# Two parts of x against the high weights in one product of 512 columns

## The reference

```
h = x @ w_in;  g = h if h > 0 else exp(h) - 1;   x = g @ w_out      # layer 0
h = x @ w_in;  g = s * max(h, 0)**2 + b;         out = g @ w_out    # layer 1
```

## Time and profile before

| | |
|---|---|
| median of 3 runs | 738.39 us (738.21 to 739.23) |
| profiled execution | 738.77 us |
| its span, first to last instruction | 736.9 us |
| PE busy | 99% of the span |
| PE weight loads | 90% |
| DVE busy | 75% |
| ACT busy | 68% |
| POOL busy | 67% |
| granted TensorE clock, mean | 0.999 |

### The profile page before, as it was taken

The page is one execution under the profiler, slowest core; times in us unless marked ns, Lnnn a source line. Parts: engine busy times, 40 slices in busy tenths (PEclk is TensorE's granted clock), DMA queues, the critical chain, the costliest instruction groups (busy, mean ns, idle before and its releaser), DMA issues.

```text
span 736.9 us, 14171 instructions
## 1 busy us (share of the span) xinstructions
PE 728.1 (99%) x4617; PEld 666.1 (90%) x4617; DVE 556.4 (75%) x1185; ACT 501.6 (68%) x941; POOL 496.5 (67%) x436
## 2 busy tenths in 40 slices
PE   8999999999999999999999999999999999999998
PEld 5999999999999889988998899989998999899986
DVE  6888888888888887877666777677767776766764
ACT  7888888888885767575657666577566656474552
POOL 6678899999998687835654577677655454644340
PEclk9999999999999999999999999999999999999999
DMA  5686765665524222321112223132112211131101
GB/s 167 160 177 134 162 169 138 156 170 123 136 61 107 86 89 85 115 58 58 31 56 59 61 88 110 58 95 85 52 57 78 78 47 58 58 102 43 58 1 57
DMA packets 78287, 67.82 MB, mean 92 GB/s; under 512 B 9284, under 2 KB 66964, under 8 KB 78228
## 3 DMA queue, kind: packets, MB, share of 16 engines
q1 hardware_dynamic: 77940, 66.80, 33.6%
q10 hardware_dynamic: 288, 0.26, 0.1%
HBM read 46.23 MB, written 3.19 MB: 67 GB/s over the span
## 4 chain that ended last, share of the span: by engine, by line
PE 79%; POOL 9%; DMA 4%; issue 4%; ACT 2%; DVE 2%; SPq 0%; POOLq 0%; DVEq 0%; ACTq 0%
PE acc L939 35%; PE h_ps L919 32%; PE pt_ps L859 4%; PE pv_ps L874 2%; PE pv_ps L875 2%; PE s_ps L845 2%; PE s_ps L846 2%; POOL pt_lo L562 2%; DMA x_parts<-x_second 2%; POOL qqk L550 1%; POOL pt_hi L560 1%; DMA qqk<-qqk 1%; POOL x L578 1%; POOL x_sum L569 1%; DMA qqk<-bits 1%
## 5 line engine op out<-in xcount | busy, mean ns | idle before, releaser
L624 POOL TENSOR_TENSOR wi_lo<-w_raw,wi_hi 128x512 fp32r<-128x512 f32 x96 | 98.8, 1030 | 188.6 <-ACT wi_hi L1035 186.0
L919 PE MATMUL h_ps<-xb_hi,wi_hi 128*128 128x256 f32 x672 | 190.2, 283 | 0.5 <-DVE u_sb L1362 0.5
L919 PE MATMUL h_ps<-xb_hi,wi_lo 128*128 128x256 f32 x672 | 190.2, 283 | 0.0
L919 PE MATMUL h_ps<-xb_lo,wi_hi 128*128 128x256 f32 x672 | 190.2, 283 | 0.0
L919 PEld LDWEIGHTS h_ps<-xb_hi,wi_hi 128*128 128x128 f32 x672 | 128.8, 192 | 2.6 <-DVE u_sb L1362 0.7
L919 PEld LDWEIGHTS h_ps<-xb_lo,wi_hi 128*128 128x128 f32 x672 | 128.8, 192 | 1.8
L919 PEld LDWEIGHTS h_ps<-xb_hi,wi_lo 128*128 128x128 f32 x672 | 128.8, 192 | 0.0
L629 POOL TENSOR_TENSOR wi_lo<-wi_sum,wi_hi 128x512 fp32r<-128x512 f32 x96 | 122.6, 1298 | 1.9 <-ACT wi_hi L1035 1.9
L1157 ACT ACTIVATE r_sb<-h_sb 128x512 f32<-128x512 f32 x96 | 60.0, 625 | 76.8 <-DVE h_sb L1379 76.8
L1217 DVE TENSOR_SCALAR_CACHE_REDUCE probs<-s_ps 128x768 f32<-128x768 f32 x96 | 91.8, 957 | 10.4 <-PE s_ps L846 7.6
L939 PE MATMUL acc<-g_hi,wo_late 128*128 128x512 f32 x288 | 91.8, 390 | 0.0
(11 more groups left out here) (122 smaller groups left out, 1676.1 us busy)
## 6 DMA issues: line engine op xcount, KB each, us to landing
w_raw<-w_in_dram SPq DMA_DIRECT2D x96, 256.0 KB, 3.1
wo_raw<-w_out_dram SPq DMA_DIRECT2D x32, 256.0 KB, 2.9
raw<-qk_dram SPq DMA_DIRECT2D x15, 384.0 KB, 5.8
qqk<-kt SPq DMA_DIRECT2D x15, 384.0 KB, 4.6
raw_v<-v_dram SPq DMA_DIRECT2D x16, 192.0 KB, 4.9
x_parts<-x_second SPq DMA_DIRECT2D x16, 192.0 KB, 6.5
qqk<-qqk SPq DMA_DIRECT2D x15, 192.0 KB, 2.8
kt<-kt SPq DMA_DIRECT2D x15, 192.0 KB, 4.6
```

The source lines that it names most:

```text
L624: return nc.gpsimd.tensor_tensor(flat(lo[:, j]), w_raw[step % 2][:, cols], flat(hi[:, j]).bitcast(F32), ALU.subtract)
L919: last = mm(h_ps[bank][:, 0:Q], w[i][:, k * P:(k + 1) * P], x[j][:, k * Q:(k + 1) * Q], start=k == 0 and m == 0, stop=k == DK - 1 and m == 2)
```

## The change

Four of the seven products (n = 0, 1, 3, 4) are made wide. For each k block the high weights meet the high and the low part of x in one matmul of 512 columns, whose result fills the whole bank: high x high in the first 256 columns, high x low in the second. The two matmuls of the low weights go to the first 256 columns as before. So such a product has 4 matmuls and not 6. What stands in the second half of the bank has to be added too, by VectorE: four more additions of 128 x 256, `P1_ALL`, a second one for U2, for U3 and for C11. Product n = 4 now waits for `P1_ALL` where it waited for ScalarE's copy. To be met in one matmul, the two parts of x become two halves of one tensor in memory, at the same addresses as before.

```diff
+WIDE = (0, 1, 3, 4)
-U2, U4, U3, C22, C11, C12, C21 = range(1, 8)
-SUMS = 7
+P1_ALL, U2_HALF, U2, U4, U3_HALF, U3, C11_HALF, C22, C11, C12, C21 = range(1, 12)
+ALL_SUMS = range(1, 12)
+SUMS = len(ALL_SUMS)
...
-        xb_hi = [xb_hi0, sb("xb_hi1", [P, 7, DK * Q], F32R)]
...
-        xb_lo = [xb_lo0, sb("xb_lo1", [P, 7, DK * Q], F32R)]
+        xb = [xb0, sb("xb1", [P, 2, 7, DK * Q], F32R)]
+        xb_hi, xb_lo = [[t[:, part] for t in xb] for part in range(2)]
...
                     if n == 4:
-                        pe.wait_ge(p1_kept, step + 1)
+                        pe.wait_ge(added, SUMS * step + P1_ALL)
...
+                    if n in WIDE:
+                        both = [xb[q % 2][:, :, b, k * Q:(k + 1) * Q] for k in range(DK)]
+                        wide = h_ps[bank][:].rearrange("p (w n) -> p w n", w=2)
+                        mm(wide, w[0][:, 0:P], both[0], start=True, stop=False)
+                        for k in range(DK):
+                            mm(h_ps[bank][:, 0:Q], w[1][:, k * P:(k + 1) * P], x[0][:, k * Q:(k + 1) * Q], start=False, stop=False)
+                        mm(wide, w[0][:, P:DK * P], both[1], start=False, stop=True).then_inc(product_done, 1)
+                        continue
...
-                bank = [h_ps[n][:, 0:Q] for n in range(HBANKS)]
+                bank, rest = [[t[:, cols] for t in h_ps] for cols in (slice(0, Q), slice(Q, 2 * Q))]
...
                 for n in part:
-                    if n == U2:
+                    if n == P1_ALL:
+                        dve.wait_ge(p1_kept, step + 1)
+                        last = tt(p1, rest[0], p1, ALU.add)
+                    elif n == U2_HALF:
                         dve.wait_ge(product_done, NP * step + 2)
-                        dve.wait_ge(p1_kept, step + 1)
-                        wait(dve, added, done - SUMS)
+                        dve.wait_ge(added, done + P1_ALL)
                         last = tt(u2, bank[1], p1, ALU.add)
+                    elif n == U2:
+                        dve.wait_ge(added, done + U2_HALF)
+                        last = tt(u2, rest[1], u2, ALU.add)
...
-                    elif n == U3:
+                    elif n == U3_HALF:
                         dve.wait_ge(product_done, NP * step + 4)
                         last = tt(u3, bank[3], u2, ALU.add)
+                    elif n == U3:
+                        dve.wait_ge(added, done + U3_HALF)
+                        last = tt(u3, rest[3], u3, ALU.add)
                     elif n == C22:
                         dve.wait_ge(added, done + U3)
+                        last = tt(h_sb[1][:, other], bank[2], u3, ALU.add)
+                    elif n == C11_HALF:
+                        dve.wait_ge(product_done, NP * step + 5)
                         wait(dve, g_made, 2 * step)
-                        last = tt(h_sb[1][:, other], bank[2], u3, ALU.add)
+                        last = tt(h_sb[0][:, first], bank[0], p1, ALU.add)
                     elif n == C11:
-                        dve.wait_ge(product_done, NP * step + 5)
-                        last = tt(h_sb[0][:, first], bank[0], p1, ALU.add)
+                        dve.wait_ge(added, done + C11_HALF)
+                        last = tt(h_sb[0][:, first], rest[0], h_sb[0][:, first], ALU.add)
```

More of the change, by code:

```diff
@@ L145, in build @@
         wo_early = sb("wo_early", [P, EARLY, 2, W], F32R)
-        xb_hi0 = sb("xb_hi0", [P, 7, DK * Q], F32R)
         over = ExitStack()
+        sb("xb_high0", [P, 7, DK * Q], F32R, over)
         xb_sum0 = sb("xb_sum0", [P, 4, DK * Q], F32, over)
         over.close()
-        xb_lo0 = sb("xb_lo0", [P, 7, DK * Q], F32R)
+        xb0 = sb("xb0", [P, 2, 7, DK * Q], F32R)
         wi_hi0 = sb("wi_hi0", [P, 7, DK * P], F32R)
@@ L217, in build @@
         r_sb = [sb(f"r_sb{n}", [P, CHUNK], F32) for n in range(2)]
-        xb_hi = [xb_hi0, sb("xb_hi1", [P, 7, DK * Q], F32R)]
+        sb("xb_high1", [P, 7, DK * Q], F32R, over)
         xb_sum = [xb_sum0, sb("xb_sum1", [P, 4, DK * Q], F32, over)]
         over.close()
-        xb_lo = [xb_lo0, sb("xb_lo1", [P, 7, DK * Q], F32R)]
+        xb = [xb0, sb("xb1", [P, 2, 7, DK * Q], F32R)]
+        xb_hi, xb_lo = [[t[:, part] for t in xb] for part in range(2)]
         g_hi = [sb(f"g_hi{n}", [P, CHUNK], F32R) for n in range(GRING)]
@@ L1421, in _ @@
                 if step == 1:
-                    sums(step, (U2, U4, U3))
+                    sums(step, range(P1_ALL, C11_HALF))
                     combine_w(2, (S1, S3))
-                    sums(step, (C22, C11, C12, C21))
+                    sums(step, range(C11_HALF, C21 + 1))
                     combine_w(2, (S2, S4))
@@ L1428, in _ @@
                 else:
-                    sums(step, (U2, U4, U3, C22, C11, C12, C21))
+                    sums(step, ALL_SUMS)
                 gate(step, 0)
```

## The result

| | before | after |
|---|---|---|
| median, us | 738.31 (6 runs) | 744.58 (6 runs) |
| ratio, 95% interval | | 1.0089 (1.0079 to 1.0100) |
| profiled execution / its span, us | 738.77 / 736.9 | 745.21 / 743.4 |

The change costs 6.3 us. The forecast was 745.8, range 740.5 to 750.5. Against the profiled execution of the kernel before (738.77) the sum said +7.4; the two profiled executions lie 6.4 apart.

The account below looks back on a forecast made before the run. PE was taken to bound steps 3 to 47, VectorE steps 0 to 2. Profiled 738.77 + 4.9 (start) + 6.8 (stalls) - 4.3 (PE's saving) = 746.2 us, less 0.4 for the median: 745.8 us, range 740.5 to 750.5.

Parts of the forecast that it names:

- What PE saves: PE's `hidden` matmuls: two of 256 columns become one of 512 eight times a step, saving 0.096 us a step.
- rival 2: The wide matmul on PE saves nothing (0.240 us), PE's step stays 10.50 us; total 748 us, chance 0.13.
- What VectorE pays: VectorE's sums with four more additions: 2.30 us from P1_ALL to U3, 3.66 us from P1_ALL to C12.
- Rings with `combine_x`: VectorE from P1_ALL to the next P1_ALL, `combine_x` included: 10.64 us in layer 0, 10.76 in layer 1, over PE's 10.41.
- Rival 3: VectorE's waits cost more, 3.84 us a step from P1_ALL to C12; total about 750 us, chance 0.12.
- rival 1: VectorE carries the added sums at 0.34 us each or less, gates unmoved; 734 or 738 to 740 us, chance 0.13.
- How late may it be: P1_ALL must start by 1.45 us after PE's first `hidden` matmul, or product 6 waits for U3; a restart costs 0.10 more.
- the slack: P1_ALL starts at 1.32 us against a limit of 1.45, leaving 0.13 us before PE stalls at product 6.
- Steps 3 to 47: Steps where PE's own time counted before: 6.8 us of new stalls against 4.3 us saved by PE.
- step 8: GpSimd subtractions hold up `combine_w` in step 7, so P1_ALL of step 8 is 1.05 us late, 1.2 with the restart.
- The three times 0.1 us for GpSimd: VectorE meets the end of a GpSimd subtraction at three places where it counts, 0.1 us of stall each.
- Steps 0 to 2: VectorE sets the end in these first steps; added sums cost 4.9 us, moving `output(1)` from 249.93 to 254.8 us.

Follow-up runs that it names:

- e2: Wide matmuls with only the seven sums of the kernel before, so the result is incomplete; 734.18 us, ratio 0.9938 to the kernel before.
- e1: Changed kernel with every matmul narrow again but all eleven sums kept; 747.58 us, ratio 1.0121 to the kernel before.
- e3_start_narrow: Changed kernel with steps 0 to 2 as in the kernel before (narrow, seven sums); 741.87 us, ratio 1.0046 to the kernel before.
- e4: Changed kernel with `combine_x` from step 2 on moved ahead of the first gate; 741.35 us, ratio 1.0041 to the kernel before.
- e8_both_all: Changed kernel with `combine_x` ahead of the first gate and steps 0 to 3 left narrow; 736.75 us, ratio 0.9976 to the kernel before.
- e7: Kernel before the change with only `combine_x` moved ahead of the first gate; 737.65 us, ratio 0.9997 to the kernel before.
- e5: Changed kernel with `combine_x` ahead of the first gate and steps 0 to 3, 5, 8, 20, 28 narrow; 734.20 us, ratio 0.9945 to the kernel before.
- e6: Changed kernel, wide only in 25 steps from 6 on not following a `combine_x` (nor step 8), `combine_x` unmoved; 735.62 us, ratio 0.9966 to the kernel before.

## Why the prediction was right

**What PE saves.** 0.096 us a step was forecast; steps that TensorE sets went from 10.50 to 10.40, and e2 gives 4.0 us for 45 such steps by the medians, 4.5 by the traces. The wide matmul with x in two pieces costs what one in one piece costs. That disposes of rival 2. By the isolated gap that the Trainium skill gives ("TensorE: Matmul & The Clock Gate", section Back-to-back issue gap) all 384 joinings would have saved 1.0 us, an estimate from that page; the runs disagree.

**What VectorE pays.** P1_ALL to the second sum of U3 2.30, as forecast; to C12 3.63 against 3.66. Rings with `combine_x`: 10.60 and 10.72 against 10.64 and 10.76; the others lie under 10.40, as their steps are TensorE's 10.40 long. Rival 3 (waits cost more) would have shown 3.84, rival 1 (VectorE carries it) 3.40.

**How late may it be.** The restart came 0.48 us after the sum it waited for and cost 0.10 more, as in the one case of the trace before. e1 tests the slack itself. With six narrow products ahead of product 6 it is 6 x 0.719 - 0.47 - 2.30 - 1.32 = 0.22 us, more than the 0.14 by which a ring of layer 0 is over 10.50: the first step behind a `combine_x` should not stall. Step 17 is 10.50 us there and 10.58 in the changed kernel, 0.18 over its 10.40. Of the whole, 747.6 was expected and 747.58 measured.

**Steps 3 to 47.** `output(1)` to `output(46)` is 729.03 - 254.32 = 474.7 us in the chain, against 45 x 10.40 = 468.0: 6.7 us of stalls, where 6.8 stood in the sum. Nearly all lie where it put them: behind a `combine_x` 0.8 us (q = 0 and 1), 1.0 us (q = 2) and 1.3 us (q = 3 and 4) a chunk, step 8 1.1 us. That the sums agree to 0.1 us is partly luck: q = 1, step 8 and the two chunks of layer 1 together came out 0.4 us lower than forecast, and the stall of step 38 (last section), which the prediction did not have, adds 0.3. The three times 0.1 us for GpSimd are mostly in the steps behind `combine_x` of q = 0 and 2. The meeting with GpSimd ahead of step 8 is the costliest of one step. Timeline after, POOL and DVE; it answers to the earlier trace rows, with P1_ALL at 314.92, where U2 stood.

```profile
311.20 2.73 POOL L696 TENSOR_TENSOR xb<-xb_sum,xb 128x512 fp32r<-128x512 f32 x2
...
311.96 0.81 DVE L1316 TENSOR_TENSOR wi_sum<-w_raw 128x256 f32<-128x256 f32 x1
312.70 1.51 DVE L1318 TENSOR_TENSOR wi_sum<-w_raw 128x256 f32<-128x256 f32 x1
...
314.92 0.42 DVE L1374 TENSOR_TENSOR p_sb<-h_ps,p_sb 128x256 f32<-128x256 f32 x1
```

Over all steps the first addition of `combine_w` is shorter than before (the 632 ns of the earlier trace rows are now 461), as VectorE comes later and meets GpSimd less (seen in step 2, under e3_start_narrow; not followed through all steps). Same view as rows 9:

```profile
L1316 DVE TENSOR_TENSOR wi_sum<-w_raw 128x256 f32<-128x256 f32 x44 | 20.3, 461 | 0.0
```

**Steps 0 to 2.** 4.8 us against 4.9: from the first sum of step 0 to that of step 1 it is 1.57 us more (forecast 1.68), to that of step 2 another 1.79 (1.78), and from there to `output(1)` 1.44 (1.44). What the prediction did not say is that in these steps product 4 waits for P1_ALL as well (three waits, 2.2 us); U3 comes later still, so it decides. Removing the start's share (e3) must give these 4.8 us less the 1.0 of the longer stall in step 3, so 3.8. From the first sum to the end of the span the trace of e3 is 4.0 us shorter than that of the changed kernel (740.3 - 229.49 against 743.4 - 228.63), but the medians differ by 2.7 only. In the profiled executions the difference lies outside that stretch: e3's has its first sum 0.9 us later, and 3.2 us of its time are outside the span, where it is 1.8 in the changed kernel's. The medians of the spans differ by 2.9. When the first sum started in the executions without a profile is not recorded, so the last 1.1 us stay open.

**What was off.** The forecast was 1.2 us too high at 745.8. The sum was 746.2 for a profiled execution, and that took 745.21. Of this 1.0 us, 0.6 is the first sum, which started at 228.63 and not at 229.20; 0.4 is in the terms (start 0.1, stalls 0.1, TensorE's saving 4.5 and not 4.3). The last 0.2 is the step from the profiled execution to the median, 0.6 and not 0.4. The first 0.6 is chance: the attention ahead ends earlier or later from one execution to the next (below). Counted from the first sum, the change costs 7.1 us in the traces, of the 7.4 of the sum. The expectation that the PE waits would list U3 some 20 times was wrong, as that view shows 5; by the distances of starts it is indeed 20 steps (3 to 5, 8 to 12, 17 to 20, 25 to 28, 33 to 36) that take 10.58 us or more, and step 38.

## What to carry to other kernels

Before trading TensorE instructions for additions, write down the other engine's ring from its first dependent instruction round to the same one of the next step, with start-to-start pitches, and hold it against TensorE's step in each kind of step; the average share (75%) says nothing. Where the ring is too long by tenths, look for a gap in it (here one of 1.0 us while ScalarE worked) before giving the change up, and apply the change only in the steps that have room: the same edit cost 6.3 us in all 48 steps and, with one addition moved into the gap, saved 3.7 us in 40 of them.

## What the runs showed that was not expected

One sum of VectorE starts 0.36 us later than its operand explains: U2_HALF should start 0.52 behind P1_ALL and starts 0.88 behind. Four of the ten traces have it, each once: in step 38 of the changed kernel, of e1 and of e4, and in step 44 of e8_both_all. It costs TensorE 0.3 us. The profile shows no cause; it stays open.

```profile
631.34 0.42 DVE L1374 TENSOR_TENSOR p_sb<-h_ps,p_sb 128x256 f32<-128x256 f32 x1 [0.18 <-ACT p_sb L1049]
632.22 0.42 DVE L1378 TENSOR_TENSOR u_sb<-h_ps,p_sb 128x256 f32<-128x256 f32 x1 [0.46 <-DVE p_sb L1374]
```

The untouched attention ends at different times: the first sum of step 0 starts at 229.20 us before, 228.63 after, 231.50 in e4 and 227.97 in e7; the changed kernel and e4 have the same code up to there. From there to `output(1)` all kernels with the added sums in steps 0 to 2 agree within 0.02 us in the chain (25.69, 25.70, 25.71), so a start's cost is better read from that point than from the span. The same holds for a whole kernel. Counted from the first sum to the last instruction, the kernel before takes 507.7 us; the changed one takes 7.1 more, e1 9.3, e3 3.1, e4 3.3, e7 0.0 (one trace each), and e2 takes 4.5 less, e5 3.7, e6 2.4, e8 1.3. The differences of the medians are up to 0.8 us off these.
